# A fused attention, expert and token/channel mixer kernel: the last expert's last slot peeled, and the mixer's first five row tiles loaded during it

## The reference

```python
# attention, B=4, heads=8, S=576, head_dim=64: pooled attention (mean over 4, repeated) + local attention (|i-j| < 4)
out = out_up + out_local                       # -> x of [4, 576, 512]
# mixture of experts, E=8, F=1024
e  = argmax(x @ w_gate)  if s == 0 or sigmoid(x @ w_local) < 0.5  else  the expert of token s-1
p  = softmax(x @ w_gate)
y[b, s] = p[e] * (relu(x[b, s] @ w1[e]) @ w2[e])
# mixer on y, d_tok=256, d_ch=1536
h  = relu(y^T @ w_tok1) @ w_tok2               # over the 576 tokens of a batch
u  = y + h^T
out = u + relu(u @ w_ch1) @ w_ch2
```

## Time and profile before

| what | value |
|---|---|
| three runs | 879.18, 881.27, 883.62 us (median 881.27) |
| the profiled execution: its time / its span | 879.94 us / 878.2 us |
| busy in the span: TensorE, its weight loads | 844.7 us (96%), 691.5 us (79%) |
| busy: VectorE, ScalarE, GpSimd | 394.0 us, 334.2 us, 216.0 us |
| mean granted TensorE clock | 0.996 of full |
| chain that ended last | TensorE 78%, VectorE 5%, GpSimd 5%, DMA 4%, issue 3%, ScalarE 3% |

### The profile page before, as it was taken

One profiled execution on the slowest core, in us unless ns is written; L12 is line 12 of the kernel. 1 busy time (PEld: TensorE's weight loads), 2 busy tenths in 40 slices (PEclk: granted clock), 3 DMA queues, 4 the chain that ended last, 5 costly groups with the idle time before them and its releaser, 6 DMA issues.

```text
span 878.2 us, 14506 instructions
## 1 busy us (share of the span) xinstructions
PE 844.7 (96%) x5137; PEld 691.5 (79%) x5138; DVE 394.0 (45%) x786; ACT 334.2 (38%) x856; POOL 216.0 (25%) x322
## 2 busy tenths in 40 slices
PE   8999898978999999999999989999999999999998
PEld 4667676645787888888788768989999889999997
DVE  4777777867452625366635364121123251221211
ACT  4677777643353525355635341111112111111110
POOL 6888888825112121211222200000000000000000
PEclk9999999998999999999999999999999999999999
DMA  9789898311646614366536140001020200000100
GB/s 167 136 129 219 171 216 191 119 54 55 209 140 205 228 52 135 140 230 190 178 116 213 48 156 1 1 5 68 1 72 1 72 0 1 1 37 1 37 1 36
DMA packets 94130, 88.49 MB, mean 101 GB/s; under 512 B 63213, under 2 KB 68991, under 8 KB 94079
## 3 DMA queue, kind: packets, MB, share of 16 engines
q1 hardware_dynamic: 87835, 74.62, 31.1%
q0 software_dynamic: 3840, 12.59, 4.3%
q10 hardware_dynamic: 2404, 0.60, 0.4%
HBM read 72.31 MB, written 15.48 MB: 100 GB/s over the span
## 4 chain that ended last, share of the span: by engine, by line
PE 78%; DVE 5%; POOL 5%; DMA 4%; issue 3%; ACT 3%; ACTq 0%; DVEq 0%; POOLq 0%; SPq 0%
PE scores L1660 11%; PE scores L1661 11%; PE scores L1662 11%; PE bank L1662 6%; PE bank L1660 6%; PE bank L1661 6%; PE bank L1712 4%; PE bank L1719 4%; PE bank L1713 4%; DMA stage<-in_moe_w 2%; POOL asb L744 2%; PE scores L1524 1%; PE bank L1448 1%; ACT asb L906 1%; PE scores L1703 1%
## 5 line engine op out<-in xcount | busy, mean ns | idle before, releaser
L1371 DVE SCALAR_TENSOR_TENSOR h2l<-scores,h2h 128x384 fp32r<-128x384 f32 x72 | 40.2, 558 | 192.2 <-ACT h2h L1030 192.2
L1030 ACT ACTIVATE h2h<-scores 128x384 fp32r<-128x384 f32 x72 | 35.4, 492 | 229.8 <-PE scores L1662 229.8
L1660 PE MATMUL scores<-uTh,W 128*128 128x384 f32 x288 | 98.1, 341 | 0.0
L1661 PE MATMUL scores<-uTl,W 128*128 128x384 f32 x288 | 97.5, 338 | 0.0
L1662 PE MATMUL scores<-uTh,W 128*128 128x384 f32 x288 | 97.3, 338 | 0.0
L1662 PE MATMUL bank<-W,h2l 128*128 128x512 f32 x216 | 84.4, 391 | 0.0
L1660 PE MATMUL bank<-W,h2h 128*128 128x512 f32 x216 | 84.3, 390 | 0.0
L1661 PE MATMUL bank<-W,h2h 128*128 128x512 f32 x216 | 84.0, 389 | 0.0
L1309 DVE TENSOR_TENSOR W<-stage,W 128x1024 fp32r<-128x1024 f32 x56 | 66.8, 1220 | 23.5 <-ACT W L976 21.0
L1712 PE MATMUL bank<-W,hTh 128*128 128x512 f32 x184 | 76.3, 415 | 0.0
L976 ACT ACTIVATE W<-stage 128x1024 fp32r<-128x1024 f32 x56 | 58.0, 1055 | 48.0 <-DVE ysb L1327 24.3
(11 more groups left out here) (236 smaller groups left out, 1646.0 us busy)
## 6 DMA issues: line engine op xcount, KB each, us to landing
stage<-in_moe_w SPq DMA_DIRECT2D x56, 512.0 KB, 4.8
vl<-in_v SPq DMA_DIRECT2D x40, 128.0 KB, 3.7
qraw<-in_q SPq DMA_DIRECT2D x32, 144.0 KB, 5.4
v<-in_v SPq DMA_DIRECT2D x8, 576.0 KB
ub<-y_dr SPq DMA_DIRECT2D x18, 256.0 KB, 4.2
out<-ob SPq DMA_DIRECT2D x18, 256.0 KB, 2.7
x_dr<-xrow SPq DMA_DIRECT2D x16, 256.0 KB, 3.7
raw<-in_moe_w SPq DMA_DIRECT2D x8, 512.0 KB, 4.9
```

The costliest lines, as they stand in the source:

```text
L1030: act.activation(dst, bank[bk][:, 0:width], ACT.Relu).then_inc(relu_hi, 1)
L1371: dve.scalar_tensor_tensor(dst, bank[bk][:, 0:width], 0.0, hi.bitcast(F32), ALU.max, ALU.subtract).then_inc(bank_free, 1)
L1660: pe.matmul(ps, ah, bh, start=first, stop=False)
L1661: pe.matmul(ps, ah, bl, start=False, stop=False)
```

## The change

The diff below is cut to its core. In it PRO is 2, NST 4, NMIX_C1 8, NK5 5 and NMIX 14.

1. **Peeled slot.** The last slot of expert 7 (`final`, a number that four new VectorE operations at the end of the routing compute together with `pair_slots`) is written out behind the loop over the expert's other slots, on TensorE, VectorE, ScalarE and GpSimd. In the peeled slot TensorE does not turn a next slot, and GpSimd does not gather one. On TensorE the loop now stands inside a conditional.
2. **Early row tiles.** SyncE loads tiles 0 to 2 once the slots that hold tokens of batches 0 and 1 have been scattered (`pair_slots`), and tiles 3 and 4 once TensorE has turned the last slot's `hs`, whose place they take. Tiles 5 to 8 still wait for `moe_done`. `ub` is nine tiles at nine places now; five low parts have places of their own (`xl0`).
3. **Mixer chunks.** Chunks 0 and 1 are split ahead of expert 7's first slot, 2 to 5 inside the peeled slot, 6 and 7 behind the five row tiles, 8 to 10 behind row tiles 5 to 8, 11 to 13 later still.
4. **TensorE.** The probabilities are turned ahead of the peeled slot and the 36 matmuls are gone. The first two `token_up` of `pr` 0 become `first_token_up`: first all 20 products that need only the high parts of the row tiles, then the 10 with the low parts. The number of matmuls is the same.

```diff
@@ SyncE
-            for m in range(NMIX_C1 + NST):
+            for m in range(PRO + NST):
+                load_mix(m)
+            early = sp.value_load(pair_slots[0:1, 0:1], min_val=E - 1, max_val=NSLOT)
+            sp.wait_ge(scattered, 16 * early)
+            for t in range(3):
+                load_y(0, t)
+            for m in range(PRO + NST, NMIX_C1):
+                load_mix(m)
+            final_ = sp.value_load(final[0:1, 0:1], min_val=E - 1, max_val=NSLOT - 1)
+            sp.wait_ge(hT_turned, 2 * final_ + 2)
+            for t in range(3, NK5):
+                load_y(0, t)
+            for m in range(NMIX_C1, NMIX_C1 + 2):
                 load_mix(m)
             sp.wait_ge(moe_done, 1)
-            for t in range(9):
+            for t in range(NK5, 9):
                 load_y(0, t)
-            for m in range(NMIX_C1 + NST, NMIX):
+            for m in range(NMIX_C1 + 2, NMIX):
                 load_mix(m)
@@ GpSimd: the peeled slot (no gather), then moe_done
+            def last_slot(j):
+                pool.tensor_copy(snow[:, :], sidx[:, bass.ds(j, 1)]).then_inc(idx_done, 1)
+                pool.wait_ge(idx_done, 2 + 2 * j)
+                pool.wait_ge(y_copied, j + 2)
+                pool.sem_inc(pool_pass, 1)
+                pool.indirect_dma_start(out=y_dr, ..., in_=ysb[:, :], in_offset=None).then_inc(scattered, 16)
+                pool.wait_ge(scattered, 16 * j + 16)
...
@@ ScalarE: slot(j, split, last)
+                if last:
+                    act.wait_ge(prob_turned, 1)
+                    act.activation(prob[:, :], bank[7][:, 0:NT], ACT.Copy).then_inc(prob_ready, 1)
                 relu(0)
+                if last:
+                    hi_mix(PRO)
                 h_hi(0)
+                if last:
+                    hi_mix(PRO + 1)
                 relu(1)
-                x_hi(j + 1)
+                if not last:
+                    x_hi(j + 1)
                 h_hi(1)
+                if last:
+                    for m in range(PRO + 2, PRO + NST):
+                        hi_mix(m)
...
+            slot(final_, None, last=True)
+            act.wait_ge(prob_ready, 1)
+            for i in range(NK5):
+                x_hi_tile(0, i)
+            for m in range(PRO + NST, NMIX_C1):
+                hi_mix(m)
             act.wait_ge(w1_free, 1)
             for pr in range(2):
                 for m in range(T1 // P):
                     h1_hi(pr, 0, m)
-                    if pr == 0:
-                        hi_mix(NMIX_C1 + NST + m)
                 for i in range(NK5, 9):
                     x_hi_tile(pr, i)
+                if pr == 0:
+                    for m in range(NMIX_C1, NMIX_C1 + 3):
+                        hi_mix(m)
                 h1_hi(pr, 1, 0)
                 u_hi(pr, 0, 0)
+                if pr == 0:
+                    for m in range(NMIX_C1 + 3, NMIX):
+                        hi_mix(m)
@@ VectorE: four operations ahead of route_done; slot(j, split, last)
+            step(dve.tensor_scalar_add(need_i[0:1, 0:1], incl[0:1, E - 1, 1:2], float(P - 1)))
+            step(dve.tensor_single_scalar(ns_i[0:1, 0:1], need_i[0:1, 0:1], 7, ALU.arith_shift_right))
+            step(tt(pair_slots[0:1, :], ns_i[0:1, 0:1], first_at[0:1, E - 1:E], ALU.add))
+            step(dve.tensor_scalar_add(final[0:1, 0:1], last_at[0:1, E - 1:E], -1.0))
...
                 h_lo(0)
+                if last:
+                    for m in range(PRO, PRO + 2):
+                        lo_mix(m)
                 h_lo(1)
-                x_lo(j + 1)
+                if not last:
+                    x_lo(j + 1)
+                if last:
+                    for m in range(PRO + 2, PRO + NST):
+                        lo_mix(m)
...
-            for m in range(NMIX_C1, NMIX_C1 + NST):
-                lo_mix(m)
-            dve.wait_ge(moe_done, 1)
             dve.wait_ge(prob_ready, 1)
             for i in range(NK5):
                 x_lo_tile(0, i)
+            for m in range(PRO + NST, NMIX_C1):
+                lo_mix(m)
@@ TensorE
+                if e is None:
+                    with pe.If(final_ - start):
+                        with pe.Fori(start, final_) as j:
+                            slot(j)
+                    pe.wait_ge(p_in, 16)
+                    pe.transpose(bank[7][:, 0:NT], probT[:, :], ident[0:NT, 0:NT]).then_inc(prob_turned, 1)
+                    slot(final_, last=True)
...
-            pe.wait_ge(p_in, 16)
-            pe.transpose(bank[7][:, 0:NT], probT[:, :], ident[0:NT, 0:NT]).then_inc(prob_turned, 1)
-            keep_busy(36, bank[3])
-            pe.wait_ge(moe_done, 1)
+            def first_token_up():
+                for m in range(T1 // P):
+                    cols = slice(m * P, (m + 1) * P)
+                    for kk in range(NK5):
+                        if m == 0:
+                            pe.wait_ge(xh_done, kk + 1)
+                        x = slice(kk * DM, (kk + 1) * DM)
+                        pe.matmul(bank[m][:, :], t1h[:, kk, cols], xh[:, x], start=kk == 0, stop=False)
+                        pe.matmul(bank[m][:, :], t1l[:, kk, cols], xh[:, x], start=False, stop=False)
+                for m in range(T1 // P):
+                    cols = slice(m * P, (m + 1) * P)
+                    for kk in range(NK5):
+                        if m == 0:
+                            pe.wait_ge(xl_done, kk + 1)
+                        mm = pe.matmul(bank[m][:, :], t1h[:, kk, cols], xl0[kk][:, :], start=False,
+                                       stop=kk == NK5 - 1)
+                    mm.then_inc(bank_full, 1)
```

More of the change, by code:

```diff
@@ L962, in x_hi, with x_hi_tile, slot @@
                 act.activation(xTh[:, :], bank[4][:, :], ACT.Copy).then_inc(xTh_done, 1)
-            def slot(j, split):
+            def x_hi_tile(pr, i):
+                act.wait_ge(y_in[i], 16 * pr + 16)
+                act.activation(xh[:, i % NK5 * DM:(i % NK5 + 1) * DM], ub[i][:, :], ACT.Copy,
+                               scale=prob[:, 9 * pr + i:9 * pr + i + 1]).then_inc(xh_done, 1)
+            def slot(j, split, last=False):
                 def chunks(lo, hi):
                     if split is None:
[L968 to L971, removed]
                         return
@@ L1024, in _ @@
                            ).then_inc(tok_hi, 1)
-            expert(E - 1, (0, None))
+            start = act.value_load(starts[0:1, E - 1:E], min_val=E - 1, max_val=NSLOT - 1)
+            final_ = act.value_load(final[0:1, 0:1], min_val=E - 1, max_val=NSLOT - 1)
+            act.wait_ge(y_copied, start + 1)
+            for m in range(PRO):
+                hi_mix(m)
+            with act.If(final_ - start):
+                with act.Fori(start, final_) as j:
+                    slot(j, None)
+            slot(final_, None, last=True)
+            act.wait_ge(prob_ready, 1)
+            for i in range(NK5):
+                x_hi_tile(0, i)
             def relu_bank(pr, dst, bk, use, width):
@@ L1293, in lo_mix, with slot @@
                 tt(lo, st, hi.bitcast(F32), ALU.subtract).then_inc(lo_done[m % 2], 1)
-            def slot(j, split):
+            def slot(j, split, last=False):
                 def chunks(lo, hi):
                     if split is None:
-                        return
-                    if split[1] is None:
-                        for m in range(lo, hi):
-                            lo_mix(m)
                         return
@@ L1360, in _ @@
             tt(t2l[:, :, up], raw2[:, :, up], t2h[:, :, up].bitcast(F32), ALU.subtract).then_inc(tok_split, 1)
-            expert(E - 1, (0, None))
+            start = dve.value_load(starts[0:1, E - 1:E], min_val=E - 1, max_val=NSLOT - 1)
+            final_ = dve.value_load(final[0:1, 0:1], min_val=E - 1, max_val=NSLOT - 1)
+            for m in range(PRO):
+                lo_mix(m)
+            with dve.If(final_ - start):
+                with dve.Fori(start, final_) as j:
+                    slot(j, None)
+            slot(final_, None, last=True)
             dve.sem_inc(bank_free, 2)
@@ L1683, in expert, with slot @@
                 w2l = wlo[par][:, KD * F:].rearrange("p (k d) -> p k d", k=KF)
[L1685 removed]
+                k = E - 1 if e is None else e
+                pe.wait_ge(hi_done, CPE * k + CPE + NST)
                 for i in range(2):
[L1687 to L1690 removed]
+                    pe.wait_ge(lo_done[i], CPE // 2 * k + (CPE + NST) // 2)
+                at_ = slice(E - 1, E) if e is None else bass.ds(e, 1)
+                start = pe.value_load(starts[0:1, at_], min_val=0, max_val=NSLOT - 1)
+                if e is None:
+                    final_ = pe.value_load(final[0:1, 0:1], min_val=E - 1, max_val=NSLOT - 1)
+                else:
+                    end_ = pe.value_load(ends[0:1, at_], min_val=1, max_val=NSLOT)
+                def slot(j, last=False):
                     def up_part(n, ks):
@@ L1728, in expert @@
                     up_part(1, [2, 3])
```

(20 more changed lines are left out.)

76 lines of the change are left out of this document (38 added, 38 removed).

## The result

| | before | after |
|---|---|---|
| median (lowest to highest) | 881.27 us (879.18 to 883.62) | 872.65 us (870.81 to 874.22), 4 runs |
| profiled execution: its time / its span | 879.94 / 878.2 us | 870.81 / 868.8 us |
| TensorE busy, VectorE, ScalarE | 844.7, 394.0, 334.2 us | 836.5, 393.8, 333.5 us |

The ratio is 0.9904, with a 95% interval of 0.9877 to 0.9932: 0.7 to 1.2% faster, as forecast (872.3 us, range 868.5 to 876.5).

What follows compares the result with a forecast made beforehand. TensorE's own stream bounds the expert stage; the gain is its delayed mixer entry. Terms: -10.6 (`token_down` earlier) + 2.0 (`turn_u` wait) + 0.1 = -8.5 us, giving 871.4 to 872.8, stated as 872.3 us; 8-in-10 range 868.5 to 876.5.

Steps and rivals of the forecast that it cites:

- Upper bound of the entry: Last slot's end to `token_down`: 6.9 us of matmuls take 18.0 us, so hiding the entry gives at most 11.1 us.
- Peeled slot: Expert 7's last slot on TensorE: transposes dropped (0.4 us), probabilities' transpose added (0.2 us); ends at about 500.6, not 500.8.
- rival 3: Stall unrelated to data, from late code fetch or a lower clock: 3.1 us lost, gain only 5.4 us, 875.9 us; chance 6%.
- Routing operations: Four more VectorE operations ahead of `route_done`, 0.8 us, hidden by 2.25 us of idle time before the first `xTl`: zero cost.
- Early tiles: Mixer's entry: tiles 0 to 2 arrive at 496.1 to 498.6; tiles 3 and 4 late by 0.3 us, bounds 0 and 1.5.
- Low parts: VectorE at the mixer's entry: five low parts of 0.7 us done by 505.1, needed at 505.2 or later; hidden.
- The relu behind `first_token_up`: Before `token_down`: only five matmuls, 1.15 us, cover a 1.3 us relu; new wait about 0.4 us, bounds 0.2 and 1.
- Start of `token_down`: First `token_down` on TensorE starts at 508.2 against 518.82, 10.6 us earlier.
- Tiles 5 to 8 and three chunks: After the last scatter: tiles, splits and `u_rows` end at 520.5; TensorE waits 2.0 us at `turn_u`, bounds 0.4 to 5.
- From `turn_u` on: `turn_u` to channel stage: 11.7 us as before plus 0.1; splits of chunks 11 to 13 hidden by 1 us.

Runs made afterwards that it cites:

- x4: Changed kernel with row tiles 0 to 4 waiting for `moe_done` and the 36 matmuls on ones put back: 882.66 us, against 879.37 us for the kernel before.
- y1: Changed kernel with VectorE's low parts of mixer chunks 8 to 10 moved behind the first `u_rows`: 871.60 us, against 881.56 us for the kernel before.
- x1: The changed kernel itself run again, nothing altered: 873.29 us, against 879.37 us for the kernel before on the same chip.
- x2: Changed kernel with the old order of products (high, low, high per row tile) in the first two `token_up`: 874.45 us, against 879.37 us before.
- y2: Changed kernel with SyncE's loads of chunks 8 and 9 moved behind those of row tiles 5 to 8: 875.62 us, against 881.56 us before.
- z1: The changed kernel itself run a third time, nothing altered: 874.45 us, against 881.03 us for the kernel before on the same chip.
- z2: Changed kernel with six more matmuls on TensorE just ahead of its wait for `u_rows`, their result overwritten: 871.83 us, against 881.03 us before.
- y3: Changed kernel with the edits of y1 and y2 together: 870.72 us, against 881.56 us for the kernel before.
- z3: Changed kernel with the edits of y1 and y2, and the first `token_up` finishing bank 0 before bank 1: 871.85 us, against 881.03 us before.

## Why the prediction was right

The mechanism and the size of the sum held: -8.5 us forecast, -7.9 us measured from slot 21's copy. That the median (872.65) lies within 0.4 us of the forecast is chance, as two profiles differ by 1.2 us before the changed stretch begins. By its steps:

- **Upper bound of the entry**, 11.1 us: unchanged; 7.9 us of it were gained. x4 shows that nothing of it comes without the early loads.
- **Peeled slot.** Forecast 0.2 us shorter. From slot 21's copy to the mixer's first product it was 12.03 us, and before to the transpose of the probabilities 12.18 (488.61 to 500.79): 0.15 us less. There is no stall inside it. At its entry TensorE lost 0.1 us behind slot 21's last group (four matmuls from 486.30, the next start at 487.30), as it did before at the loop's end (499.79, 500.79); rival 3 had put a code fetch there.
- **Routing operations.** Hidden: VectorE's next splits began 0.9 us later (204.70 and 205.57), the idle time before `xTl` shrank from 2.25 us to 1.58 us, and `xTl` came only 0.2 us later; it waits for ScalarE in both.
- **Early tiles.** Slot 21's scatter had landed by 491.7, SyncE's issue. That is 2.8 us after its start; the 0.4 us that I gave SyncE were not there. Counted from the copy, tiles 3 and 4 were issued 0.6 us later than reckoned (496.49 against 497.1 - 1.2), the first of these landed 4.4 us later, and TensorE lost 0.8 us before tile 3, against 0.3 forecast, inside the bounds of 0 to 1.5.
- **Low parts.** Five in 3.40 us, done at 503.6, asked for at 505.2. Hidden.
- **The relu behind `first_token_up`.** 0.40 us of idle time, as forecast. (The profile counts it from the modelled end of the matmul before; from start to start 0.6 us are lost.)
- **Start of `token_down`.** Forecast 10.6 us earlier, measured 9.5 us from the common point. The 1.1 us are tile 3 (0.5), three matmuls behind its pause that started 0.34 us apart (0.3), the relu (0.2) and the others at 0.232 us, not 0.229 (0.1). They cost nothing in the end: they came out of the wait at `turn_u`.
- **Tiles 5 to 8 and three chunks.** This was the step with the widest bounds, and it alone sets the time. The scatter took 4.46 us, not the 3.1 to 3.7 that I took, and SyncE's issue followed within 0.2 us instead of 0.5 to 1.1; the two errors cancelled in part. All in us from slot 21's copy: first issue 18.3 against 17.7 forecast, last low part done 25.4 against 24.8, splits done 29.2 against 28.5, `u_rows` done 32.4 against 31.9. So `turn_u` came 0.7 us later than forecast, which is the 0.6 us that the sum is off. The wait is nevertheless shorter than the 2.0 us forecast (1.24 us idle, 1.4 from start to start), because TensorE reached it 1.2 us later than forecast; that is luck, not a term got right. In two other profiles the wait was 1.9 us. ScalarE did not quite run ahead: VectorE's first split waited 0.27 us for it. y1 shows that the splits make the wait.
- **From `turn_u` on.** 11.73 us, forecast 11.8.

What the forecast missed beyond this is in rival 3. It had a chance of 6% and was argued away with a single row, the 1.86 us wait that left the clock at 1.00. x1 shows the same kernel losing 1.5 us behind a wait of 1.93 us, and the clock falling where the prediction had called that a sign of being wrong. So rival 3 is no alternative to the forecast but an addition that comes in some of the executions. How often stays open: only one profile of each run shows where the clock fell.

## What to carry to other kernels

Loading a later stage's input as soon as its own rows are written, rather than when the whole stage is done, was worth everything here. The new order of the products was not needed for it (x2), and whether the peeled slot is needed no run tests: none has the early loads without it. When a wait is hidden, follow the rest of the dependent chain: it came back one barrier later (`u_rows`), and work that can wait should then stand behind that barrier. Where that work needs buffers that are reloaded, look at the loads too (y1, y2). And to compare two traces within a fraction of a per cent, count from the last event that the edit doesn't touch.

## What the runs showed of the hardware

- The run-to-run spread of this kernel is partly the granted clock outside the changed stretch. The slowest profiled execution of the changed kernel (x1, 875.8 us span, mean clock 0.986) was already 4.6 us late at slot 21's copy, and 4.2 us late at the first slot's (233.33 against 229.10). Its attention stage has a stretch at the low clock; the same 10 us have 1.00 in the first profile. TensorE was busy only 1.04 of the 2 us just before:

```profile
148.00:150.00 2.00, 1.04 (x11) 0.90 (x10) 0.94 (x3) 2.00 (x8) 1.67 (x4) 1.00 1.22 197
150.00:160.00 10.00, 10.00 (x80) 6.75 (x78) 4.26 (x12) 6.22 (x26) 6.61 (x7) 0.56 0.71 215
```

- z1 was as late at slot 21's copy (492.06) without that stretch. Its clock was 0.76 from 190 to 200, and at the first slot's copy it was 1.4 us late (230.50); where the rest of its lateness comes from stays open.
- Waits of 1.86 and 1.96 us (z1, x2) left the clock at 1.00, waits of 1.93 and 2.73 us (x1, y2) were followed by 0.50 to 0.77. The length of the wait alone does not decide.
- The last scatter landed 2.75 us after its start with little else in flight. With two chunk loads of 512 KB issued 3 to 4 us before it, it took 3.60 to 4.66 us in six profiles (4.46, 4.50, 4.66, 3.60, 3.64 and 4.41 in the changed kernel, x1, x2, y1, z1 and z2); without them 3.12 and 3.13 us (y2; y3 and z3). So the same loads cost it between 0.5 and 1.5 us.
